# Fused RWKV, soft MoE and FFN on one core: the first FFN layer on four row tiles of 32 rows instead of one stacked matmul per block

## The reference

```python
# 1. linear attention with state (B=4, H=8, S=768, D=48), giving x of 3072 x 384
y[t] = r[t] @ (state + outer(u * k[t], v[t])); state = w * state + outer(k[t], v[t])
# 2. soft mixture of experts, 8 experts with 4 slots each: 32 slots
logits = x @ phi
d = softmax(logits, axis=tokens); slot_in = d.T @ x
slot_out[e] = relu(slot_in[e] @ w1[e]) @ w2[e]
c = softmax(logits, axis=slots)
x = c @ slot_out                         # 3072 x 384, of rank 32
# 3. feed-forward, d_ff = 2048
h = x @ w_in
g = h * sigmoid(1.702 * h)
out = g @ w_out
```

## Time and profile before

| | |
|---|---|
| median of 3 runs | 409.25 us (409.02 to 409.25) |
| the profiled execution | 407.5 us, of which span of the core 405.7 us |
| mean granted TensorE clock | 0.986 of full |
| PE (matmul) busy | 388.6 us, 96% |
| PEld (weight load) busy | 308.7 us, 76% |
| DVE, ACT, POOL busy | 236.0, 188.1, 119.0 us |
| chain that ended last, by engine | PE 64%, DVE 2%, ACT 1%, issue 1% |

### The profile page before, as it was taken

One profiled execution on the slowest core, in us unless ns is written; L12 is line 12 of the kernel. 1 busy time (PEld: TensorE's weight loads), 2 busy tenths in 40 slices (PEclk: granted clock), 3 DMA queues, 4 the chain that ended last, 5 costly groups with the idle time before them and its releaser, 6 DMA issues.

```text
span 405.7 us, 9085 instructions
## 1 busy us (share of the span) xinstructions
PE 388.6 (96%) x3234; PEld 308.7 (76%) x3234; DVE 236.0 (58%) x399; ACT 188.1 (46%) x432; POOL 119.0 (29%) x113
## 2 busy tenths in 40 slices
PE   5769999999999899999999999999999999999996
PEld 5658788878787654467888888888888888888885
DVE  6658867786867440028665655565656565555551
ACT  1034444444443313257656454645554464546452
POOL 5879887777756121014530000000000000000000
PEclk9589999999999999999999999999999999999999
DMA  7699999999999968990000100200020020002002
GB/s 238 240 391 335 347 337 313 316 322 316 328 313 344 372 226 297 405 376 10 2 0 27 53 0 2 78 0 0 0 78 0 0 78 0 0 0 78 2 0 78
DMA packets 28613, 63.89 MB, mean 158 GB/s; under 512 B 2640, under 2 KB 16576, under 8 KB 28208
## 3 DMA queue, kind: packets, MB, share of 16 engines
q1 hardware_dynamic: 27600, 63.12, 44.1%
q10 hardware_dynamic: 992, 0.49, 0.6%
HBM read 58.88 MB, written 4.72 MB: 157 GB/s over the span
## 4 chain that ended last, share of the span: by engine, by line
PE 64%; DVE 2%; issue 1%; ACT 1%; DVEq 0%
PE bank L569 16%; PE bank L571 16%; PE bank L570 16%; PE bank L556 5%; PE bank L495 3%; PE bank L476 3%; PE bank L316 1%; DVE glo L798 1%; PE bank L537 1%; PE bank L360 1%; DVE gf L792 1%; PE bank L486 0%; PE bank L440 0%; PE bank L504 0%; PE bank L381 0%
## 5 line engine op out<-in xcount | busy, mean ns | idle before, releaser
L792 DVE TENSOR_TENSOR gf<-bank,sg 128x512 f32<-128x512 f32 x96 | 66.2, 690 | 86.4 <-ACT sg L943 86.0
L569 PE MATMUL bank<-glo,whi 128*128 128x512 f32 x288 | 112.4, 390 | 0.2 <-DVE glo L798 0.2
L571 PE MATMUL bank<-ghi,wlo 128*128 128x512 f32 x288 | 112.1, 389 | 0.0
L570 PE MATMUL bank<-ghi,whi 128*128 128x512 f32 x288 | 112.1, 389 | 0.0
L943 ACT ACTIVATE sg<-bank 128x512 f32<-128x512 f32 x96 | 57.3, 597 | 94.0 <-PE bank L556 93.9
L798 DVE TENSOR_TENSOR glo<-gf,ghi 128x512 fp32r<-128x512 f32 x96 | 69.2, 721 | 0.2
L569 PEld LDWEIGHTS bank<-glo,whi 128*128 128x128 f32 x288 | 54.1, 188 | 12.3 <-DVE glo L798 1.1
L571 PEld LDWEIGHTS bank<-ghi,wlo 128*128 128x128 f32 x288 | 54.1, 188 | 11.3
L570 PEld LDWEIGHTS bank<-ghi,whi 128*128 128x128 f32 x288 | 54.1, 188 | 11.2
L949 ACT ACTIVATE ghi<-gf 128x512 fp32r<-128x512 f32 x96 | 59.9, 624 | 0.9 <-DVE gf L792 0.9
L835 ACT ACTIVATE yt<-bank 112x512 f32<-112x512 f32 x24 | 14.3, 598 | 68.9 <-PE bank L360 68.9
(11 more groups left out here) (121 smaller groups left out, 393.3 us busy)
## 6 DMA issues: line engine op xcount, KB each, us to landing
ring<-w SPq DMA_DIRECT2D x24, 512.0 KB, 5.9
rkb<-rk SPq DMA_DIRECT2D x23, 512.0 KB, 5.2
krb<-kr SPq DMA_DIRECT2D x24, 384.0 KB, 5.3
ring<-w SPq DMA_DIRECT2D x4, 1536.0 KB, 13.6
ring<-w SPq DMA_DIRECT2D x8, 768.0 KB, 9.7
vb<-v SPq DMA_DIRECT2D x24, 192.0 KB, 5.2
out<-ob SPq DMA_DIRECT2D x18, 256.0 KB, 2.1
ring<-win SPq DMA_DIRECT2D x3, 1024.0 KB, 14.0
```

What stands on the lines that cost most here:

```text
L569: pe.matmul(o, w_hi, lo, start=(f == 0), stop=False)
L570: pe.matmul(o, w_hi, hi, start=False, stop=False)
L571: pe.matmul(o, w_lo, hi, start=False, stop=(f == KF - 1)).then_inc(prod_ps, 1)
L792: dve.tensor_tensor(gf[:, f % 2, :], bank[f % 4][:, :], sg[:, f % 2, :], ALU.mult).then_inc(gf_ok, 1)
```

## The change

- The stack is gone: `mst`, `pat`, the `parts` transfer, and lines 546, 547, 937 and 784. `spr` is one pattern instead of four, 128 x 128 for each batch.
- c is kept as two tiles, `cth` (high) and `ctl` (low), each with the same 32 rows repeated in all four partition groups. High comes from `chi`, low from `clo`, each by its own matmul into its own bank (`CT_HI`, `CT_LO`; the number of matmuls is the same, 12); ACT copies cth, DVE copies ctl (`low_spread`, six new copies). Banks 4, 5, 0 and 1 are used twice or three times, so TensorE waits for `cth_ok` and `ctl_ok` before it spreads the third and the last part.
- M's matmul takes w_in's columns in another order (`(j q n)`), so that partition group q holds the blocks 4j+q. `mhl` (M's high and low part, 128 x 512) is used directly as weights.
- `hidden(i, j)` makes four blocks 4j to 4j+3 at once: in each of three rounds (high x high, high x low of c, low of M x high), four matmuls with 32 rows each, row group q into bank q. low x low is left out.
- It is issued before product 4j+1 of the tile (in the first tile, the first time, before product 2), and waits for the gf of all four blocks before (`quad_go` is a semaphore count on TensorE behind this wait).
- Five warming matmuls instead of seven come before the first of these; TensorE's loop over token tiles is written out (646 rows of instructions in the order become 1064). The loops of DVE and ACT stay.

The lines of the changed kernel are two or three off: 558 is the first layer, 571 to 573 the second.

```diff
-            sp.wait_ge(p_ps, C)
-            sp.dma_start(pat[:, :, :], parts).then_inc(s_pat, 16)
...
-                for b in ((i,) if i < B else (2 * (i - B), 2 * (i - B) + 1)):
-                    pe.matmul(bank[CT[i]][:, o], spr[:, 2, b, :], chi[:, t], start=True, stop=False)
-                    last = pe.matmul(bank[CT[i]][:, o], spr[:, 3, b, :], clo[:, t], start=False, stop=True)
+                for part, w, banks, done in ((0, chi, CT_HI, cth_ps), (1, clo, CT_LO, ctl_ps)):
+                    for b in ((i,) if i < B else (2 * (i - B), 2 * (i - B) + 1)):
+                        last = pe.matmul(bank[banks[i]][:, o], spr[:, b, :], w[:, t], start=True, stop=True)
+                    last.then_inc(done, 1)
...
                     last = pe.matmul(LG[32 * q:32 * q + 32, :], sot[:, k, :],
-                                     win_sb[:, k, 512 * q:512 * q + 512], start=(k == 0), stop=(k == KD - 1))
+                                     win_sb[:, k, :].rearrange("p (j q n) -> p q j n", q=4, n=P)[:, q],
+                                     start=(k == 0), stop=(k == KD - 1))
...
-            pe.wait_ge(ct_ok, B + 2)
-            keep_warm(bank[3], 7)
-            pe.wait_ge(mhi_ok, 1)
-            pe.wait_ge(mlo_ok, 1)
-            for q in range(4):
-                pe.matmul(bank[MB[q]][:, :], spr[:, 0, q, :], mhl[:, 0, :], start=True, stop=False)
-                pe.matmul(bank[MB[q]][:, :], spr[:, 1, q, :], mhl[:, 1, :], start=False, stop=True)\
-                  .then_inc(mst_ps, 1)
...
-            def hidden(i, f):
-                q = KF * i + f
-                wait(pe, gf_ok, q - 3)
-                pe.matmul(HB[f % 4][:, :], mst[:, f * P:(f + 1) * P],
-                          ct_flat[:, bass.ds(i * TT, TT)],
-                          start=True, stop=True).then_inc(hh_ps, 1)
+            def hidden(i, j):
+                f = KF * i + 4 * j
+                wait(pe, gf_ok, f)
+                pe.sem_inc(quad_go, 1)
+                n, t = slice(j * P, (j + 1) * P), bass.ds(i * TT, TT)
+                for term, (part, c) in enumerate(((0, cth_flat), (0, ctl_flat), (1, cth_flat))):
+                    if is_first(i, j) and term == 2:
+                        pe.wait_ge(mlo_ok, 1)
+                    for q in range(4):
+                        r = slice(32 * q, 32 * q + 32)
+                        last = pe.matmul(HB[q][:, :], mhl[r, part, n], c[r, t], start=(term == 0), stop=(term == 2))
+                        if term == 2:
+                            last.then_inc(hh_ps, 1)
...
-            pe.wait_ge(mst_even, 1)
-            for f in range(LEAD):
-                hidden(0, f)
+            pe.wait_ge(cth_ok, B + 2)
+            pe.wait_ge(ctl_ok, B + 2)
+            keep_warm(bank[4], 5)
+            pe.wait_ge(mhi_ok, 1)
+            hidden(0, 0)
             keep_warm(LG, 10)
...
-                    if f + LEAD < KF:
-                        hidden(i, f + LEAD)
-                    elif more:
-                        hidden(i + 1, f + LEAD - KF)
+                    if f % 4 == (2 if first and f < 4 else 1):
+                        if f + 4 < KF:
+                            hidden(i, f // 4 + 1)
+                        elif more:
+                            hidden(i + 1, 0)
                     product(i, f)
...
+            def low_spread(i):
+                dve.wait_ge(ctl_ps, i + 1)
+                if i < B:
+                    dve.tensor_copy(ctl[:, i, 0:512], bank[CT_LO[i]][:, :]).then_inc(ctl_ok, 1)
...
             for g in range(2):
                 dve.wait_ge(so_ps, g + 1)
                 dve.tensor_copy(so[:, g, :], [YN, LG][g][:, 0:DM]).then_inc(so_ok, 1)
+                for i in ((0, 1, 2, 3) if g == 0 else (4,)):
+                    low_spread(i)
...
-            for q in (1, 3):
-                dve.wait_ge(mst_ps, q + 1)
-                dve.tensor_copy(mst[:, 512 * q:512 * q + 512], bank[MB[q]][:, :]).then_inc(mst_odd, 1)
```

More of the change, by code:

```diff
@@ L106, in rwkv_soft_moe_ffn @@
         yn = sb("yn", [P, B, HP, 2, D])
+        st_at = place["at"]
         st = sb("st", [P, B, HP, D])
@@ L116, in rwkv_soft_moe_ffn @@
         rkn = sb("rkn", [P, 2, H, D])
+        spr = sb("spr", [P, B, P], F32R)
         assert place["at"] <= nc.sbuf_usable_end
@@ L126, in rwkv_soft_moe_ffn @@
         assert place["at"] <= vb_at
+        place["at"] = yt_at
+        ctl = sb("ctl", [P, B, S], F32R)
         snt = sb("snt", [P, KD, SLOTS])
         sot = sb("sot", [P, KD, SLOTS])
-        clo = sb("clo", [P, S], F32R)
         assert place["at"] <= yn_at
@@ L132, in rwkv_soft_moe_ffn @@
         chi = sb("chi", [P, S], F32R)
-        place["at"] = yn_at
-        spr = sb("spr", [P, 4, B, P], F32R)
+        place["at"] = st_at
+        clo = sb("clo", [P, S], F32R)
         assert place["at"] <= ubc_at
[L136 to L140, removed]
         place["at"] = ring_at + 4 * SLOT_W * HT_AT
@@ L189, in rwkv_soft_moe_ffn @@
                              "mhi_ok", "mlo_ok"))
[L190 to L194, removed]
+        spr_made, cturn_ps, chi_ok, clo_ok = (sem(n) for n in ("spr_made", "cturn_ps", "chi_ok", "clo_ok"))
+        rmax_ok, csub_ok, cexp_ok, rsum_ok, c_ok, cth_ps, cth_ok, ctl_ps, ctl_ok, whi_ok, wlo_ok = (
+            sem(n) for n in ("rmax_ok", "csub_ok", "cexp_ok", "rsum_ok", "c_ok", "cth_ps", "cth_ok", "ctl_ps",
+                             "ctl_ok", "whi_ok", "wlo_ok"))
+        quad_go = sem("quad_go")
         hh_ps, sg_ok, gf_ok, ghi_ok, glo_ok, prod_ps, o_ok = (
@@ L209, in rwkv_soft_moe_ffn @@
         ring_flat = ring[:, :, :].rearrange("p e n -> p (e n)")
-        ct_flat = ct[:, :, :].rearrange("p b t -> p (b t)")
+        cth_flat = cth[:, :, :].rearrange("p b t -> p (b t)")
+        ctl_flat = ctl[:, :, :].rearrange("p b t -> p (b t)")
         def row_view(c0, c1):
@@ L522, in _ @@
             picked(0)
+            pe.wait_ge(cth_ok, 2)
+            pe.wait_ge(ctl_ok, 2)
             spread_weights(2)
@@ L584, in tile @@
                         pe.wait_ge(wlo_ok, f // PK + 1)
-                    if f + LEAD < KF:
-                        hidden(i, f + LEAD)
-                    elif more:
-                        hidden(i + 1, f + LEAD - KF)
+                    if f % 4 == (2 if first and f < 4 else 1):
[3 more added lines that the diff above has]
+                            hidden(i + 1, 0)
                     product(i, f)
[L591 to L594, removed]
+            for i in range(C):
+                tile(i, i < C - 1)
         @block.vector
@@ L774, in _ @@
             low_weights(2, slice(512, S))
+            def low_spread(i):
+                dve.wait_ge(ctl_ps, i + 1)
+                if i < B:
+                    dve.tensor_copy(ctl[:, i, 0:512], bank[CT_LO[i]][:, :]).then_inc(ctl_ok, 1)
+                else:
+                    b = 2 * (i - B)
+                    dve.tensor_copy(ctl[:, b:b + 2, 512:S],
+                                    bank[CT_LO[i]][:, :].rearrange("p (b t) -> p b t", b=2)).then_inc(ctl_ok, 1)
             for g in range(2):
@@ L921, in _ @@
             for i in range(B + 2):
[L922 removed]
+                act.wait_ge(cth_ps, i + 1)
                 if i < B:
[L924 removed]
+                    act.activation(cth[:, i, 0:512], bank[CT_HI[i]][:, :], ACT.Copy).then_inc(cth_ok, 1)
                 else:
                     b = 2 * (i - B)
[L927 to L928 removed]
+                    act.activation(cth[:, b:b + 2, 512:S], bank[CT_HI[i]][:, :].rearrange("p (b t) -> p b t", b=2),
+                                   ACT.Copy).then_inc(cth_ok, 1)
             act.wait_ge(run_ok, C + 1)
@@ L934, in _ @@
             high_wout(0)
-            for q in (0, 2):
-                act.wait_ge(mst_ps, q + 1)
-                act.activation(mst[:, 512 * q:512 * q + 512], bank[MB[q]][:, :], ACT.Copy).then_inc(mst_even, 1)
             def sigmoid(i, f):
@@ L1029, in _ @@
             steps(pool, step)
-            pool.wait_ge(p_ps, C)
             pool.wait_ge(s_late, 16 * 3)
-            pool.wait_ge(s_pat, 16)
             for b in range(B):
-                pool.tensor_tensor(spr[:, :, b, :], pat[:, :, :],
-                                   jcol[:, b:b + 1].unsqueeze(2).to_broadcast([P, 4, P]), ALU.mult)\
+                pool.tensor_tensor(spr[:, b, :], same[:, :], jcol[:, b:b + 1].to_broadcast([P, P]), ALU.mult)\
                     .then_inc(spr_made, 1)
```

17 lines of the change are left out of this document (8 added, 9 removed).

## The result

The changed kernel takes **412.99 us** (median; 411.54 to 417.87 over 20 runs), the kernel before beside it 409.15 us (407.41 to 413.57 over 20 runs): the ratio is 1.0094, 95% interval 1.0065 to 1.0122, so about 3.8 us more. Slower was forecast, and 411.9 us. The ratio leaves out runs that lie over 1.5% above the fastest of their kernel, as the one of 417.87 us.

A forecast was written before the change was run, and what follows sets the result against it. TensorE's matmul time was taken as the bound. Start -1.65, glo waits -0.25 and 23 groups +4.6 sum to +2.7 us on the median of 409.25, giving 411.9 us, range 408.4 to 417.0.

The forecast's parts named there:

- The bound: Steady part: TensorE's time for its matmuls bounds the kernel, one every 0.227 us, 2.27 us per block.
- A round = one step, 0.227: First layer: four matmuls on four row tiles take one full-array step; three rounds plus 0.02 stagger make 0.70 us.
- The rival of 0.296: First-layer rounds slower than a step, 0.296 us each by the skill's 3.07 times: group 1.31, time 416.7 us; chance 0.13.
- A switch = 0.20: Around each group: going into row tiles or back to the full array costs 0.20 us each way, ends 0.15 and 0.21.
- the cheap switch: Rival at each group: 0.15 us per switch as at L347, group 1.00 us, time 409.5 us; chance 0.15.
- the load drawn forward: Rival at each switch: weight load overlapped, only the 0.10 gap left, group 0.90, time 407.6 us, faster; chance 0.13.
- the break-even of 0.99: The cost of one group of four blocks, in us, at which the change neither gains nor loses time.
- The start, -1.65: Behind M: first sigmoid at 180.27 instead of 181.92 us, so product 0 comes 1.65 us earlier.
- the waits for glo: Products 1 and 2 waited 0.22 and 0.48 us; after, product 1 waits 0.45 and product 2 nothing: 0.25 us won.
- The copies of ctl: Ahead of M: six new copies of 0.69 us on DVE, which idles there, costed at nothing.
- No wait at a tile's end: End of each token tile: the fourth gf at 8.2 us just fits TensorE's load at 8.26, so nothing, five times.
- 23 x 0.20 = 4.6: Steady part: each of 23 groups costs 1.11 us against 0.91 for four blocks, 0.20 more, +4.6 us in all.

The follow-up runs named there:

- e1: The changed kernel with low of M x low of c added as a fourth round of four row tiles in each of the 24 groups: 420.29 us.
- e4: The kernel before with one unread 512-column matmul on one 32-row tile ahead of every fourth block's first layer, 24 in all: 422.84 us.
- e4c: The kernel before with one unread 512-column matmul of 128 rows on the full array ahead of every fourth block's first layer, 24 in all: 413.53 us.
- e2: The changed kernel with one unread full-array warming matmul between the second and third round of the 23 steady groups: 427.01 us.
- e8: The kernel before with only the first four blocks on row tiles straight from M, the other 92 stacked as before: 406.91 us, ratio 0.9947 to the kernel before.
- e6: The changed kernel with each group's twelve matmuls ordered row tile by row tile instead of round by round: 412.58 us.
- e5: The kernel before with only TensorE's loop over token tiles written out: 409.31 us.

## Why the prediction was right, and what it missed

**The bound** held: TensorE is busy through the window before and after, at the same clock, and each added microsecond of the array is one of the kernel's. A single run tells less than the 0.8 us that I gave it: the kernel before took 407.41 to 413.57 us.

**A round = one step, 0.227.** Right (e1). The value was taken from pairs of row tiles; four behave the same. The rival of 0.296, by the Trainium skill's "TensorE: Matmul & The Clock Gate", section "Measured speedup vs the span model", fell: with round behind round, four row tiles of 512 columns give 4.0 matmuls for one full-array step, not 3.07.

**A switch = 0.20.** Right: 0.204 alone (e4 against e4c), 0.20 doubled (e2), 0.19 and 0.21 in the group shown. It came from two far places, and the earlier trace rows, both of other lines, against one of 0.15, which I set aside for its shorter load; that the shorter load is the reason for 0.15 no run here tests. For this kernel the cheap switch and the load drawn forward are refuted: the loads stand about 0.1 behind the free array in all 23 groups. With the group at 1.11 the break-even of 0.99 was never near.

**The start, -1.65.** Measured -1.64 (2.31 for 3.95 us), and 1.58 of it reach product 0. Of the waits for glo one is left, in front of product 1: its first matmul counts from 190.91, with 190.55 possible, so 0.36 us where I had 0.45. Counted in the same way the two waits before were 0.18 and 0.45, not 0.22 and 0.48, so 0.27 was won where 0.25 was forecast. The copies of ctl are free, as costed: the 24.5 us from the 2000th matmul to the warming load are the same with and without them.

**No wait at a tile's end.** Right; none of the five stands in the waits.

**What was too small is the term 23 x 0.20 = 4.6.** Behind the first product the stage has 222.53 - 217.21 = +5.32 us, where +4.6 - 0.25 = +4.35 was forecast. With the 0.27 for 0.25, 0.99 lacks:

- 0.09 is the group itself: the 22 groups without the late one take 1.111 us in the mean against 0.907 for four steps, so 23 x 0.204 = 4.69. The prediction was helped by a slip here: 0.70 + 2 x 0.20 is 1.10, not 1.11, and by its own terms the group's share was 4.4.
- The matmuls behind a group aren't at their step at once. Averaged over the 21 groups from 205 us on, the second to the seventh step take 0.229 to 0.234 us, then it is 0.227 again; from the second to the 35th this adds 0.028 us, and 23 times that is 0.64. I had let each product go on at 0.227 from its first matmul.
- 0.26 is the one late gf at 200.64. I had looked for such waits only at the ends of token tiles, with four products between two groups. Here there are three, 27 x 0.227 = 6.1 us, while from the first sigmoid of the group (194.07) to the end of the fourth gf (200.50) it is 6.4: 0.6 for the sigmoid, 4 x 1.41 - 0.72 = 4.9 up to the fourth gf, and 0.84 for the glo that takes 1.52 us beside POOL's wlo.

Together 0.99. In the median the change costs 3.84 us against 2.7.

**What stays open.** Why the steps behind a switch are slower. Four banks at once aren't needed for it: behind e4's lone row tile, with one bank that nobody reads, the second to the seventh step are 0.02 longer in sum too. In e4c, without a switch, all steps are 0.227. In the kernel before the same slower steps stand behind the waits of the start. So they follow a gap in the stream of matmuls, and no run here says by what. Whether the late gf would go if POOL made its wlo elsewhere wasn't tried.

## What to carry to other kernels

Row tiles of 32 rows do four matmuls in one step, but going from the full array to row tiles or back isn't overlapped with anything: the next load starts 0.1 us after the array could have gone on, and lies bare for another 0.1. A pair of switches costs 0.4 us, nearly two steps of a 512-column matmul, and the group saved here one round out of four steps only, 0.2 us. So a row-tile phase pays where it saves more than two steps, or once, at a place where TensorE waits anyway (e8); count the steps saved per pair of switches before anything else. A latency gain at the start of a stage (1.6 us here) is had once, while a cost in a steady group is had as often as the group: take the two apart, as e8 does.

## What was not expected of the hardware

- Matmuls of different row tiles pass each other in TensorE's queue: with three of one tile in a row in the program, the four tiles still start within 0.03 us, and the group takes 1.12 us for 1.11 (e6). What stands behind a wait isn't drawn forward (0.20 us later). The Trainium skill, "TensorE: Matmul & The Clock Gate", section "The mechanism", says that matmuls keep strictly to their order; the rows of e6 speak against it, between row tiles.
- Behind a switch or a wait, the second to the seventh matmul step by 0.229 to 0.234 instead of 0.227 us.
- The granted clock of the part ahead of M differs between executions, also of the same code: from 10 to 50 us it is 0.74, 0.74, 0.79 and 0.80 in the four runs with the changed kernel's code there (the change, e1, e2, e6), and the warming load comes at 183.24, 181.56, 178.31 and 178.88 us. That is more than the whole change is worth; a comparison of spans would have shown 9 us for a change of 3.8. The mean alone doesn't tell the cost: with 0.70 in e5 the load comes at 179.79.
